# RWKV attention, gated feed-forward and top-2 experts on one core: gate columns computed with the gates as weights in four array quarters, ScalarE's copies and the router's waits in another order

## The chip, the cores and the metric

The kernel runs as one program on one core of a Trainium2 chip. The metric is the time of one execution on the device in microseconds (us), and lower is better. TensorE (PE in the rows) multiplies matrices, VectorE (DVE) and ScalarE (ACT) work on vectors, GpSimd (POOL) issues the indirect transfers and SyncE (SP) nearly all the others. Each engine has its own instruction stream and works it off in order. An engine waits for another by a semaphore.

## What is computed

Three layers in a row, all in fp32:

```python
for t in range(S):                       # B=4, H=8, S=768, D=48
    cur = einsum('bhd,bhe->bhde', u[None] * kt, vt)
    y[:, :, t] = einsum('bhd,bhde->bhe', rt, state + cur)
    state = wt[:, :, :, None] * state + einsum('bhd,bhe->bhde', kt, vt)
x = y.transpose(0, 2, 1, 3).reshape(3072, 384)
x = ((x @ w1) * (x @ w2)) @ w3 @ w_out   # w1, w2: 384x1024, w3: 1024x1024, w_out: 1024x384
noisy = x @ w_gate + log1p(exp(x @ w_noise)) * noise      # 8 experts
top2 = the two largest of noisy; weights = softmax over them
out = sum over the two of weight * (relu(x @ w1[e]) @ w2[e])
```

## The kernel before

Attention goes in chunks of 128 steps; one **pair** is two heads of one batch element, and there are 16 pairs. A pair's steps are: `in` 0 to 2 (PE transposes w, k and r into the tile `tr`, L162; ScalarE copies them out as `wt`, `kt`, `rt`, L232), `derive` (VectorE: running products `decay` L247, their reciprocals L258, `kdiv` L265, `rdec` L271), `diag` (VectorE, L282, L289, L298), `spread` (ScalarE copies the identity, scaled by the diagonal, into `att`, twelve copies of 128x128, L311), `score` (PE L177 into `pp`; VectorE masks it into `att`, L319), `keys` (PE L186, ScalarE L238), `state` (PE L198; VectorE L328 and L333), `scale` (ScalarE makes `state`, L345) and `out` (PE L217 and L223; ScalarE L352). The second `score` needs the mask of the first, since both use `pp`.

The program has four stretches. In the first, the **build** (to 115 us), pairs 0 to 3 run between the steps of a product of weights: `w_out` is transposed (`wo_turn`, L649), its product with the two gate matrices is made (`wo_gates`, L658: 48 records with `woT` as the weights and the 16 gate columns as the moving side), and w3 is transposed block by block (`w3_turn`, L669, ScalarE evacuates to `w3T`, L571) and multiplied with [w_out | gates] (`w3_mm`, L679). ScalarE and VectorE also split w1 and w2 into a high and a low part there (L583, L628), and the products (L586, L614). The second stretch, the **main** one (to 460 us), runs the other 12 pairs between the steps of the feed-forward: `up` (PE L781 into two banks in turn; ScalarE copies one half, `a_sb` L826, VectorE multiplies, `ab_all` L859, then `abh` L822 and `abl` L852; `up` number f+2 needs the `ab_all` of f), `down` (PE L797, ScalarE `x2s` L837), `turn` (the next tokens, `xh` L469 and `xl` L475), and the router: `route` in parts 0 to 3 and `place`, on VectorE with an Exp and a Ln on ScalarE (L843, L845, each Ln and the Exp of `gap`, L848, with an ACT_TABLE_LOAD ahead). The third (to 580 us) ends the feed-forward and starts the experts; the fourth is the experts' visits (L1189, L1205, L1230, L1248), whose code is not touched.

The order of the steps is one list for all engines. `pair_slots` gives ten slots for each pair; `threaded` fills the main steps in behind each slot so that each gets an equal share of the sum of their `LENGTH`s. Each engine runs through that list and issues what it has to do at each step, SP its loads too. In `pair_slots` the copy of the states (`scale`) stands ahead of `in` 0 of the next pair in slot 2, the spreads are two steps of six copies in slots 6 and 7, and `derive` 4 and 5 are in slots 7 and 8.

Before the list starts SP issues a fixed set of loads, among them the second block of w3, `load_w3(1)`.

## Time and profile before

| | us |
|---|---|
| median of three runs | 1058.26 |
| lowest and highest | 1055.92, 1060.39 |
| the profiled execution | 1058.37 |
| its span | 1056.5 |
| PE busy in it | 1018.5 |
| VectorE busy | 706.4 |
| ScalarE busy | 587.4 |

The profiled execution lies 0.11 us above the median, and 1.9 us of its time are outside the span. A row of a timeline is: start, duration, engine, line, operation, what it writes and reads, how many in a row, and in brackets the idle time of the engine before it with what ended it.
### The profile page before, as it was taken

Reading aid. Unit: us, or ns where it says so; the run is one execution under the profiler, and the core shown is the slowest. Engines: PE = TensorE matmul, PEld = TensorE weight load, DVE = VectorE, ACT = ScalarE, POOL = GpSimd, SP = SyncE. Lnnn points to the kernel's source line nnn. Section 1 sums busy time; section 2 is a strip of 40 time slices with the busy share of each in tenths; the row PEclk is TensorE's granted clock in tenths of the full one; section 3 lists DMA queues with packets and bytes.
Section 4 is the critical chain, followed back from the end, with each engine's and each line's share of the span. In section 5 each row is a group of like instructions: output and inputs, shape, how many; then the busy total and the mean of one; then the engine's idle time right before and its main releaser. Section 6 shows DMA issues by size and latency. Waiting matters only on the chain.

```text
span 1056.5 us, 20547 instructions
## 1 busy us (share of the span) xinstructions
PE 1018.5 (96%) x7791; PEld 957.0 (91%) x7791; DVE 706.4 (67%) x1339; ACT 587.4 (56%) x1125; POOL 222.2 (21%) x209
## 2 busy tenths in 40 slices
PE   7999999999999999999998999999999999999995
PEld 6666789989899988999998999999999999999995
DVE  5878567778688677735677658565775857576570
ACT  4655456456456455533564557565664756566471
POOL 0000000110110110111214332343234233323321
PEclk8999999999999999999999999999999999999998
DMA  9654432553634733120557979787888978888851
GB/s 248 168 147 92 105 81 62 84 119 67 88 70 81 119 59 51 43 87 16 185 118 135 270 201 303 208 252 233 237 258 221 291 212 252 247 225 270 225 157 16
DMA packets 190886, 166.41 MB, mean 158 GB/s; under 512 B 118258, under 2 KB 174452, under 8 KB 190788
## 3 DMA queue, kind: packets, MB, share of 16 engines
q1 hardware_dynamic: 177012, 144.76, 50.1%
q0 software_dynamic: 12976, 20.32, 9.8%
q8 instruction: 62, 1.02, 0.4%
q14 instruction: 36, 0.29, 0.1%
q10 hardware_dynamic: 800, 0.02, 0.0%
HBM read 141.21 MB, written 25.22 MB: 158 GB/s over the span
## 4 chain that ended last, share of the span: by engine, by line
PE 90%; ACT 3%; DVE 2%; DMA 2%; issue 1%; POOL 0%; another core or an unknown queue 0%; SPq 0%; DVEq 0%; ACTq 0%; POOLq 0%
PE bank L1189 18%; PE pp L1205 18%; PE bank L781 18%; PE fx L797 10%; PE tr L162 3%; PE yu L1248 3%; PE pp L177 2%; PE yu L223 2%; PE yu L217 2%; PE fx L679 2%; PE bank L679 2%; PE tr L1170 2%; PE yu L1230 1%; PE fx L1230 1%; DMA slot_entry<-entry,slot_i 1%
## 5 line engine op out<-in xcount | busy, mean ns | idle before, releaser
L781 PE MATMUL bank<-xh,w12h 128*128 128x256 f32 x576 | 167.0, 290 | 4.3 <-DVE ab_all L859 3.7
L781 PE MATMUL bank<-xl,w12h 128*128 128x256 f32 x576 | 162.8, 283 | 0.0
L781 PE MATMUL bank<-xh,w12l 128*128 128x256 f32 x576 | 162.7, 282 | 0.0
L1103 POOL DMA_INDIRECT result<-x2s,who x55 | 93.2, 1695 | 275.0 <-ACT x2s L1322 249.9
L1309 DVE SCALAR_TENSOR_TENSOR abl<-bank,abh 128x512 fp32r<-128x512 f32 x96 | 66.2, 690 | 109.9 <-ACT abh L1304 101.7
L958 POOL DMA_INDIRECT slot_entry<-entry,slot_i x48 | 50.0, 1041 | 379.7 <-DVE token_f L947 368.4
L781 PEld LDWEIGHTS bank<-xh,w12h 128*128 128x128 f32 x576 | 110.1, 191 | 7.3 <-DVE ab_all L859 5.0
L781 PEld LDWEIGHTS bank<-xl,w12h 128*128 128x128 f32 x576 | 110.3, 191 | 0.0
L781 PEld LDWEIGHTS bank<-xh,w12l 128*128 128x128 f32 x576 | 110.1, 191 | 0.0
L1189 PE MATMUL bank<-xh,set_up_h 128*128 128x256 f32 x384 | 109.2, 284 | 0.2 <-DVE abl L1309 0.2
L1189 PE MATMUL bank<-xh,set_up_l 128*128 128x256 f32 x384 | 108.6, 283 | 0.0
L1189 PE MATMUL bank<-xl,set_up_h 128*128 128x256 f32 x384 | 108.6, 283 | 0.0
L1304 ACT ACTIVATE abh<-bank 128x512 fp32r<-128x512 f32 x96 | 57.4, 598 | 84.5 <-PE bank L1189 80.6
L859 DVE TENSOR_TENSOR ab_all<-a_sb,bank 128x256 f32<-128x256 f32 x96 | 40.3, 420 | 76.3 <-ACT a_sb L826 71.0
L1205 PE MATMUL pp<-set_down_h,abh 128*128 128x384 f32 x256 | 87.7, 342 | 0.0
L1090 POOL DMA_INDIRECT xr<-ffn_out,who x55 | 74.9, 1362 | 59.0 <-DMA who<-slot_entry 33.2
L1205 PE MATMUL pp<-set_down_h,abl 128*128 128x384 f32 x256 | 85.7, 335 | 0.0
L1205 PE MATMUL pp<-set_down_l,abh 128*128 128x384 f32 x256 | 85.6, 334 | 0.0
L826 ACT COPY a_sb<-bank 128x256 f32<-128x256 f32 x96 | 35.2, 367 | 88.2 <-PE bank L781 84.4
L258 DVE RECIPROCAL kdiv<-decay 128x256 f32<-128x256 f32 x48 | 82.9, 1738 | 0.2
L1322 ACT ACTIVATE x2s<-pp,who 128x384 f32<-128x384 f32 x48 | 27.9, 582 | 85.0 <-PE pp L1205 80.5
L1189 PEld LDWEIGHTS bank<-xh,set_up_h 128*128 128x128 f32 x384 | 73.5, 191 | 0.7 <-DVE abl L1309 0.4
(233 smaller groups left out, 2762.2 us busy)
## 6 DMA issues: line engine op xcount, KB each, us to landing
up_raw<-in_moe_w SPq DMA_DIRECT2D x93, 512.0 KB
down_raw<-in_moe_w SPq DMA_DIRECT2D x124, 384.0 KB
padded<-in_w SPq DMA_DIRECT2D x32, 144.0 KB, 2.8
padded<-in_k SPq DMA_DIRECT2D x32, 144.0 KB
padded<-in_r SPq DMA_DIRECT2D x32, 144.0 KB
vs<-in_v SPq DMA_DIRECT2D x32, 144.0 KB, 3.5
attention_out<-yt SPq DMA_DIRECT2D x64, 72.0 KB, 1.9
xr<-attention_out SPq DMA_DIRECT2D x12, 384.0 KB, 3.7
```

The source lines that it names most:

```text
L258: nc.vector.reciprocal(kdiv[q % 2][:, :].rearrange("p (c x) -> p c x", c=NC)[:, two, :], decay[q % 2][:, two, 1:C + 1]).then_inc(inverse_r ...
L679: last = nc.tensor.matmul(sums[q % 2][:, 0:WA], w3T[q % 2][:, m, :], wo[:, m, :], start=(m == 0), stop=(m == KF - 1))
L781: last = nc.tensor.matmul(bank[f % 2][:, m * TG:(m + 1) * TG], wp[:, m, kk, f * P:(f + 1) * P], xp[:, kk, :], start=(n == 0), stop=(n == 3 ...
L797: last = nc.tensor.matmul(fx[:, 0:WA], xp[:, f, s * P:(s + 1) * P], wp[:, f, :], start=(f == 0 and n == 0), stop=(f == KF - 1 and n == 2))
L859: nc.vector.tensor_tensor(ab[f % 4], a_sb[f % 2][:, :], bank[f % 2][:, TG:2 * TG], ALU.mult).then_inc(ab_free, 1)
L958: nc.gpsimd.indirect_dma_start(slot_entry, bass.IndirectOffsetOnAxis(slot_i[:, s, n:n + 1], 0), entry[:, s, n, :], None).then_inc(scattere ...
L1090: nc.gpsimd.indirect_dma_start(xg[v % 2][:, s, :], None, stored, bass.IndirectOffsetOnAxis(who[v % 4][:, s, 0:1], 0)).then_inc(gathered[v ...
L1103: nc.gpsimd.indirect_dma_start(out, bass.IndirectOffsetOnAxis(who[v % 4][:, s, 0:1], 0), yo[v % 2][:, s, 0:DM], None, bounds_check=N - 1, ...
L1189: last = nc.tensor.matmul(bank[m % 2][:, f * T2:(f + 1) * T2], wp[:, kk, c:c + P], xp[:, kk, :], start=(n == 0), stop=(n == 3 * KD - 1))
L1205: last = nc.tensor.matmul(pp[:, s, 0:DM], xp[:, f, s * P:(s + 1) * P], wp[:, f, :], start=(f == 0 and n == 0), stop=(f == KF - 1 and n == 2))
L1304: nc.scalar.activation(hh[:, 2 * m:2 * m + 2, :].rearrange("p a t -> p (a t)"), bank[m % 2][:, :], ACT.Relu).then_inc(hh_ready, 1)
L1309: nc.vector.scalar_tensor_tensor(hl[:, 2 * m:2 * m + 2, :].rearrange("p a t -> p (a t)"), bank[m % 2][:, :], 0.0, hh[:, 2 * m:2 * m + 2, : ...
```

## The change

1. `wo_gates` becomes one step. The gates, padded with zeros from 16 to 32 columns (a memset on GpSimd, `gates_clear`), are the weights, and `woT` is the moving side, 256 columns at a time: twelve matmuls, three for each quarter of 32 columns of the array. ScalarE copies the 128x256 result into `w3T[1]`, a new step `gates_turn` transposes it back with two transposes on PE, and VectorE copies that into `wo`. In the list `w3_turn` 0,1 stands between the two steps. `LENGTH` gets `gates_turn` 1, while three `wo_gates` of 5 are gone.
2. The spreads are four steps of three copies, at the slots that `SPREAD_AT` names for each pair (5 to 9). The first two parts need only that the first half of the previous output is done. The mask waits for the two parts of its half.
3. In slot 2 `in` 0 stands ahead of `scale`, and `derive` 4 and 5 are both in slot 7.
4. `route` part 0 ends before the wait for the Ln, which goes with its three operations to part 1. The wait for the Exp of `gap`, with the two operations behind it, goes to a part 4, called at the start of `place`.

```diff
+        SPREAD_AT = ((5, 6, 8, 9), (5, 7, 8, 9), (5, 6, 7, 9), (6, 7, 8, 9))
...
-                    [("scale", q, 0), ("in", q + 1, 0)],
+                     [("in", q + 1, 0), ("scale", q, 0)],
...
-                    [("derive", q + 1, 3), ("spread", q + 1, 0)],
-                    [("derive", q + 1, 4), ("spread", q + 1, 1)],
-                    [("derive", q + 1, 5)], []]
+                     [("derive", q + 1, 3)], [("derive", q + 1, 4), ("derive", q + 1, 5)], [], []]
...
-            build += [("wo_gates", n, 0) for n in range(4)] + [("w3_turn", 0, 1)]
+            build += [("wo_gates", 0, 0), ("w3_turn", 0, 1), ("gates_turn", 0, 0)]
...
+                        for kk in range(KD):
+                            for n in range(4):
+                                last = nc.tensor.matmul(fx[4 * E * n:4 * E * (n + 1), 0:2 * P], gates[:, kk, :],
+                                                        woT[:, kk, 2 * P * n:2 * P * (n + 1)],
+                                                        start=(kk == 0), stop=(kk == KD - 1))
...
+                elif part == 1:
                     dve.wait_ge(ln_ready, i + 1)
...
-                else:
+                elif part == 3:
...
-
+                else:
                     dve.wait_ge(exp_ready, 2 * i + 2)
...
             def dve_place(dve, b, q):
 
                 i = NG * b + q
+                dve_route(dve, b, q, 4)
                 dve.wait_ge(place_full, i + 1)
```

PE's instructions at the start, from the transposes of w_out to the first output of pair 0. Before:

```order
L669 MATMUL bank<-ident,w3r 128x128 x4
L162 MATMUL tr<-ident,padded 128x128 x6
L658 MATMUL fx<-gates,woT 128x16 x24
L177 MATMUL pp<-rdec,kdiv 128x128 x6
L186 MATMUL tr<-ident,kdiv 128x128 x5
L669 MATMUL bank<-ident,w3r 128x128 x4
L177 MATMUL pp<-rdec,kdiv 128x128 x6
L198 MATMUL yu<-vs,kend_t 64x48 x10
L669 MATMUL bank<-ident,w3r 128x128 x4
L679 MATMUL fx<-wo,w3T 128x400 x2
```

and of the changed kernel (its L685 is L669 of before, its L695 is L679):

```order
L685 MATMUL bank<-ident,w3r 128x128 x4
L162 MATMUL tr<-ident,padded 128x128 x6
L670 MATMUL fx<-woT,gates 32x256 x12
L685 MATMUL bank<-ident,w3r 128x128 x4
L677 MATMUL fx<-ident,w3T 128x128 x2
L685 MATMUL bank<-ident,w3r 128x128 x4
L695 MATMUL fx<-wo,w3T 128x400 x4
L177 MATMUL pp<-rdec,kdiv 128x128 x6
L186 MATMUL tr<-ident,kdiv 128x128 x5
L177 MATMUL pp<-rdec,kdiv 128x128 x6
L198 MATMUL yu<-vs,kend_t 64x48 x10
```

The first transposes of the second w3 block (the third L685 row) and four matmuls of `w3_mm` moved ahead of the scores L177, and nothing stands between L186 and the second scores.

ScalarE in the build, from the transposed r of pair 2 to its keys. Before:

```order
L232 COPY rt<-tr 128x768
L586 CAST wah<-fx 128x400
L311 ACTIVATE att<-ident,diag 128x128 x12
L571 COPY w3T<-bank 128x512
L583 CAST w12h<-wraw 128x1024
L571 COPY w3T<-bank 128x512
L238 COPY kend_t<-tr 128x640
L586 CAST wah<-bank 128x400
L345 ACTIVATE state<-added,decay 128x48 x5
L232 COPY wt<-tr 128x768
```

and of the changed kernel (L313 is L311, L578 is L571, L593 is L583, L596 is L586, L347 is L345):

```order
L232 COPY rt<-tr 128x768
L313 ACTIVATE att<-ident,diag 128x128 x3
L578 COPY w3T<-bank 128x512
L313 ACTIVATE att<-ident,diag 128x128 x3
L593 CAST w12h<-wraw 128x1024
L313 ACTIVATE att<-ident,diag 128x128 x3
L578 COPY w3T<-bank 128x512
L313 ACTIVATE att<-ident,diag 128x128 x3
L596 CAST wah<-bank 128x400
L238 COPY kend_t<-tr 128x640
```

The first copy out of the w3 transposes now stands behind three spread copies in place of twelve. The copy of `wt` and the states follow a few rows on, with `wt` first.

VectorE in the main stretch, at part 0 of the route of a group. Before:

```order
L258 RECIPROCAL kdiv<-decay 128x256
L886 TENSOR_SCALAR one_z<-exp_z 128x16
L887 SCALAR_TENSOR_TENSOR rest<-one_z,exp_z 128x16
L889 RECIPROCAL noisy<-one_z 128x16
L890 TENSOR_TENSOR rest<-rest,noisy 128x16
L892 TENSOR_TENSOR rest<-ln_z,rest 128x16
L893 TENSOR_TENSOR rest<-rest,noise_all 128x16
L895 TENSOR_TENSOR noisy<-rest,x2s 128x16
L859 TENSOR_TENSOR ab_all<-a_sb,bank 128x256
L852 TENSOR_TENSOR abl<-ab_all,abh 128x256
L265 TENSOR_TENSOR kdiv<-kt,kdiv 128x768
```

and of the changed kernel (L875 is L859, L868 is L852, L909 is L892):

```order
L902 TENSOR_SCALAR one_z<-exp_z 128x16
L903 SCALAR_TENSOR_TENSOR rest<-one_z,exp_z 128x16
L905 RECIPROCAL noisy<-one_z 128x16
L906 TENSOR_TENSOR rest<-rest,noisy 128x16
L875 TENSOR_TENSOR ab_all<-a_sb,bank 128x256
L868 TENSOR_TENSOR abl<-ab_all,abh 128x256
L265 TENSOR_TENSOR kdiv<-kt,kdiv 128x768
L271 TENSOR_TENSOR rdec<-rt,decay 128x768
L875 TENSOR_TENSOR ab_all<-a_sb,bank 128x256
L868 TENSOR_TENSOR abl<-ab_all,abh 128x256
L909 TENSOR_TENSOR rest<-ln_z,rest 128x16
```

The operation that waits for the Ln moved behind two `ab_all`, and `rdec` moved up to `kdiv`.

## Rows read from the trace of the kernel before

**Rows 1.** The page, part 4: the chain that ended last, by engine.
```profile
PE 90%; ACT 3%; DVE 2%; DMA 2%; issue 1%; POOL 0%; another core or an unknown queue 0%; SPq 0%; DVEq 0%; ACTq 0%; POOLq 0%
```

**Rows 2.** What PE waited for: us in total, times, the longest.
```profile
PE tr L162 <- ACT wt L232: 6.0, 6, 1.5
...
PE bank L781 <- DVE ab_all L859: 3.7, 5, 1.0
...
PE pp L177 <- issue: 1.8, 2, 0.9
```

**Rows 3.** Stretches: length, busy time of each engine, PEclk, DMA share, GB/s.
```profile
19.70:26.50 6.80, 6.80 (x40) 6.21 (x40) 1.95 (x3) 1.97 (x5) 0.00 (x0) 0.50 0.91 244
...
67.50:70.90 3.40, 3.40 (x9) 2.03 (x9) 2.79 (x3) 0.69 (x1) 0.00 (x0) 0.50 0.91 239
```

**Rows 4.** The timeline of PE in the first 50 us.
```profile
15.68 6.60 PE L658 MATMUL fx<-gates,woT 128*128 128x16 f32 x48
...
27.77 0.66 PE L669 MATMUL bank<-ident,w3r 128*128 128x128 f32 x4
...
31.61 0.82 PE L162 MATMUL tr<-ident,padded 128*128 128x128 f32 x6
...
32.79 0.65 PE L217 MATMUL yu<-rdec,state 48*64 48x128 f32 x8
33.38 0.88 PE L223 MATMUL yu<-att,vs 128*64 128x128 f32 x12
...
39.83 2.85 PE L679 MATMUL bank<-wo,w3T 128*128 128x400 f32 x8
...
44.39 0.94 PE L177 MATMUL pp<-rdec,kdiv 48*128 48x128 f32 x12
45.26 0.77 PE L186 MATMUL tr<-ident,kdiv 128*128 128x128 f32 x5
...
48.17 0.79 PE L198 MATMUL yu<-vs,kend_t 128*64 128x48 f32 x20
```

**Rows 5.** The load of w3's second block that SP issues at 18.16 us.
```profile
L510 SPq DMA_DIRECT2D w3r<-in_moe_w x1: 542/542/542, 18.2 to 18.2; - x1
...
DMA to landing us min/median/max: 5.4/5.4/5.4
```

**Rows 6.** Timelines of VectorE, ScalarE and PE: the first mask, and pair 2 in the build.
```profile
23.98 1.01 DVE L319 COPY_PREDICATED att<-causal,pp 128x768 f32<-128x768 int32 x1 [1.37 <-PE pp L177]
...
61.82 3.61 ACT L311 ACTIVATE att<-ident,diag 128x128 f32<-128x128 f32 x12
...
65.96 0.66 PE L669 MATMUL bank<-ident,w3r 128*128 128x128 f32 x4 [1.43 <-ACT w3T L571]
```

**Rows 7.** The timeline in the main stretch where states stand ahead of `wt`.
```profile
211.37 1.49 ACT L345 ACTIVATE state<-added,decay 128x48 f32<-128x48 f32 x5 [1.80 <-DVE added L328]
...
212.77 0.78 ACT L232 COPY wt<-tr 128x768 f32<-128x768 f32 x1
...
213.69 0.85 PE L162 MATMUL tr<-ident,padded 128*128 128x128 f32 x6 [1.45 <-ACT wt L232]
...
216.62 0.65 PE L217 MATMUL yu<-rdec,state 48*64 48x128 f32 x8
```

**Rows 8.** The timeline at the Ln of a route, second batch element.
```profile
286.72 1.75 DVE L258 RECIPROCAL kdiv<-decay 128x256 f32<-128x256 f32 x1
...
288.20 1.28 ACT L845 ACT_TABLE_LOAD   x1
...
289.82 0.18 DVE L892 TENSOR_TENSOR rest<-ln_z,rest 128x16 f32<-128x16 f32 x1 [0.62 <-ACT ln_z L845]
...
290.92 0.39 PE L781 MATMUL bank<-xh,w12h 128*128 128x256 f32 x1 [1.00 <-DVE ab_all L859]
```

**Rows 9.** The timeline of VectorE behind the Exp of `gap`.
```profile
260.40 0.17 DVE L920 TENSOR_SCALAR total<-exp_gap 128x2 f32<-128x2 f32 x1 [0.68 <-ACT exp_gap L848]
...
261.48 0.95 DVE L271 TENSOR_TENSOR rdec<-rt,decay 128x768 f32<-128x768 f32 x1
```

**Rows 10.** The chain that ended last, around the scatter of the last but one group.
```profile
554.61 12.37 DMA slot_entry<-entry,slot_i
```

More of the change, by code:

```diff
@@ L576, in first_act @@
                         evacuate(q)
+                    elif step == "wo_gates":
+                        act.wait_ge(gates_full, 1)
+                        nc.scalar.copy(w3T[1][:, 0:2, :].rearrange("p n f -> p (n f)"), fx[:, 0:2 * P]).then_inc(gates_out, 1)
                     elif step == "w3_turn":
```

67 lines of the change are left out of this document (37 added, 30 removed).

## The prediction

> **What bounds the kernel now.** I read the chain that ended last first: PE carries 90% of it [rows 1]. So only three things count: work that leaves PE, idle time of PE, and time at the low clock. The list of what PE waited for gives the second: 6.0 us for ScalarE's copy of `wt` in six places, 3.7 us for `ab_all`, 1.8 us at the scores [rows 2]. The stretches give the third: from 19.7 to 26.5 and from 67.5 to 70.9 us PE was granted 0.50 and was busy all the time [rows 3]. The first of these began inside the gate step, 48 records in 6.6 us [rows 4].
>
> **The gate step and the start.** The change takes 48 records away that are paced by their loads of weights. In their place come 24 records of 256 columns and two transposes. No row shows four quarters. Two halves are in the trace: twelve records of 128 columns in 0.88 us [rows 4], 0.073 us each, so 0.147 for 256 columns and 3.5 us for 24. Without any overlap a record costs what the full array needs: 2.85 us for eight of 400 columns [rows 4], 0.89 ns a column, 5.5 us in all. With all four quarters beside each other it is near 1.4 us. So PE is done with the gates between 17.1 and 21.2 us, and behind `w3_turn` 0,1 and the transposes between 18.4 and 22.3. None of this reaches the end. The next steps in the list are now the transposes of w3's second block. SP issues its load at 18.16 us and it lands 5.4 us later, at 23.6 [rows 5]; the order of SP up to there is not changed, and its queue is full of earlier loads. Before, these transposes ran at 27.77 [rows 4] and met no wait. Now PE stands still 1 to 5 us in front of them, and the scores, which need nothing from that load, are queued behind.
>
> What is left from 23.6 on: before, from 27.77 to 32.79 us is 5.0 us [rows 4], of which two transposes of inputs (0.82 us each, 0.65 from start to start) don't count, since they come later in the new list as well: 3.7. Added are two scores, the keys and the state products, 0.94 + 0.94 + 0.77 + 0.79 [rows 4], 3.1 us with their overlaps. Nothing stands any more between the keys and the second scores, so these wait for the mask of the first: 1.01 us [rows 6] and 0.2 to start it, less the 0.6 of the keys, 0.6 us. Together 7.4 us, which ends at 31.0. The same point of before is 32.79 - 1.3 = 31.5. At full clock the start gains 0.5 us.
>
> But the clock. In the build an idle of 1.43 us [rows 6] and the light work behind it were followed by 3.4 us at 0.50 [rows 3]. I take one such piece behind the new, longer idle: 3.4 us at half rate lose 1.7. The start then **loses 1.2 us**. Bounds: a gain of 0.5 if the gates run without overlap, the idle is short and the clock stays; a loss of 2.9 if the low piece is as long as the first one, 6.8 us [rows 3].
>
> The Trainium skill has a rule that speaks against this change (TensorE: Matmul & The Clock Gate, "HAM oscillation — how this bites in real kernels"): if the array has to wait for a transfer between two stretches of matmuls, it is throttled and begins the next stretch cold. By that rule the wait for w3 costs a cold stretch; without it my sum would be 1.7 us lower. The trace agrees as far as it goes, with an idle that a copy caused and not a transfer.
>
> **Spreads in four parts.** In pair 2 the copy out of the w3 transposes stands behind twelve spread copies of 3.61 us [rows 6]. In the new order it stands behind three, 0.9 us. PE's idle of 1.43 us goes, and with it the low piece behind it, 1.7 us: **-3.1 us**. What is late next is VectorE: by my count of the steps it has some 12 us of work from `wt` to `rdec`, and PE 13 to 14 us between the same two points, so it fits, with about 1 us to spare. One of the build's pairs gets the keys and second scores side by side, which costs 0.6 us for the mask as above: **+0.6**.
>
> **`wt` ahead of the states.** ScalarE waited 1.80 us for VectorE's `added` and then made the states, 1.49 us; the `wt` copy came behind and PE idled 1.45 us for it [rows 7]. Now the copy starts when its transposes have ended, and these stand ahead of VectorE's work on the states; it is done before PE wants `tr`. All six waits go: **-6.0 us** [rows 2]. The states are up to 0.8 us later. The output that reads them starts at 216.62 [rows 7], 3.8 us behind the last state; that covers it. The bound is -3: in the build the shares between steps are short, and a wait may come back there.
>
> **The route's waits.** In three places PE idled 1.00 us for `ab_all` [rows 8]. The chain there: reciprocal of 1.75 us on VectorE, `one_z` behind it, ScalarE's table load of 1.28 us and Ln, `a_sb`, and VectorE's wait of 0.62 for the Ln with three small operations, before `ab_all` [rows 8]. The new order takes the Ln's wait and the three operations (0.6 us) away, and three of the six spread copies in front of the Exp. I work the new times out: reciprocal to 288.5, `one_z` to 288.6, Ln to 288.8, `a_sb` to 289.1, `ab_all` to 289.8. PE wants it at 289.92. So the idle just goes, with 0.1 us to spare: -3.0, and -0.2 in the last route: **-3.2 us**. Where the last spread part now stands right in front of the Exp, the next `up` but one comes 4 us later, behind the scores, so nothing waits.
>
> `rdec` at 261.48 [rows 9] came behind the wait for the Exp of `gap`, and the scores waited 0.9 us for it, twice [rows 2]. It now follows `kdiv` at once and ends 2 us earlier: **-1.8 us**. The gap, its Exp and the following `ab_all` are 0.6 us later, behind a `down` that has 1.7 us in hand.
>
> In the last groups two operations (0.4 us) are now part of `place`, ahead of the scatter whose transfer of 12.37 us is in the chain [rows 10]. The late table hangs on it, and PE is idle behind that table: **+0.4 us**. In the other groups nothing waits for `place`. From 580 us on the code and the order are the same, and I expect the same time. GpSimd's memset of the gates lies beside the first loads, at no cost.
>
> **Sum.** Against the profiled execution, 1058.4: -6.0 - 3.1 - 3.2 - 1.8 = -14.1; +1.2 + 0.6 + 0.4 = +2.2. That is -11.9: **1046.5 us**. The profiled execution stands at the median, so I take the same for the median.
>
> **The rivals.**
> *B: the waits of the route come back in another form.* My margin at the Ln is 0.1 us, and the reciprocal in front of `one_z` stays where it is. For it: VectorE has next to no idle time in such a group. Against it: the spread copies in front are halved. If half a microsecond more is late in each of the places, and the states or VectorE give back as much as one wait for each batch element, 4 to 5 us of the gain stay away: 1051.
> *C: the start and the build take more back.* The low piece is 6.8 us long (+1.7), and VectorE's margin of under 1 us in the build breaks in two or three pairs (+2), on top of half of B (+2.3): 1052.5 to 1054, within half a per cent of before.
> *D: slower than before.* One mechanism: after the wait for w3 the clock stays low through the build, because the small waits for masks there keep it from rising. Work at half rate costs 0.5 us for each us. The gains outside the start are 13.1 - 0.4 us or so; from some 25 us of low clock on, up to about 49 us in the run, it is a loss. If it lasts through the 90 us of the build, +45 - 13: 1090. Against it: before, the clock rose again inside 7 us each time [rows 3], among work as light as this.
> That the change doesn't do what it says is true for its first part in my forecast already: the gate columns are shorter on PE and the end doesn't see it.
>
> **How the numbers follow.** Forecast 0.63, its own range 1043.5 to 1049 (the start from -0.5 to +2.9 in place of +1.2, the finale's 0.4 or not, a build wait more or less). B 0.19 at 1051, C 0.13 at 1053, D 0.05. The range that holds 8 in 10 reaches over B: 1043 to 1054. A difference of 0.5%, 5.3 us, is about what a measurement of this kernel can tell from no change; faster than 1053.0 are the forecast, B and half of C: 0.88; within it 0.07; slower 0.05.
>
> **What would show it.** PE idle 1 to 5 us in front of the third w3 transposes, ending near 23.6 us, and PEclk at 0.50 behind it. No wait for `wt`, none for `w3T` behind spreads, no low clock near 68 us. The wait of VectorE for the Ln gone, `rdec` straight behind `kdiv`. The main stretch some 8 us shorter, the build from 30 us on some 4. I am wrong if PE has no idle near 20 us (then the start gains 1 to 3 us more), if the idle of 1.00 us is still there three times, or if PE waits for state copies, `kend_t` or masks in the main stretch.

## The result, and the profile after

The changed kernel takes **1053.2 us** in the median of 19 runs (1049.5 to 1056.0), beside 1060.0 for the kernel before on the same chip (19 runs): a ratio of **0.9938**, 95% interval 0.9925 to 0.9951. The medians are 6.8 us apart where 11.9 were forecast. Three more comparisons, one on chip 1 and two on chip 2, gave 0.9921, 0.9959 and 0.9968. Lines have moved by 16 below the diff, and by 17 behind `place`: L781 is now L797, L797 is L813, L810 is L826, L669 is L685, L1189 is L1206.

What PE waited for in the changed kernel, without the first load of all and the rows under 1.1 us (us in total, times, the longest), from its profiled execution of 1054.0 us:

```profile
PE bank L685 <- DMA w3r<-in_moe_w: 5.3, 1, 5.3
...
PE yu L223 <- issue: 3.4, 1, 3.4
PE fx L813 <- ACT x2s L853: 3.1, 8, 0.7
PE bank L1206 <- DVE abl L1326: 2.5, 2, 2.0
PE tr L162 <- ACT wt L232: 1.2, 2, 0.6
PE bank L826 <- DVE abl L1326: 1.1, 1, 1.1
PE bank L797 <- DVE ab_all L875: 1.1, 1, 1.1
```

Against [rows 2], `wt` fell from 6.0 to 1.2 us, the route's waits at `ab_all` from 3.7 to 1.1 (that one is in the last groups), and the 1.8 us at the scores are gone. Of the long rows two are new. The first is the wait for w3's second block, as forecast. This is the timeline of PE there:

```profile
15.11 1.50 PE L670 MATMUL fx<-woT,gates 128*32 128x256 f32 x24
16.55 0.66 PE L685 MATMUL bank<-ident,w3r 128*128 128x128 f32 x4
17.11 0.44 PE L677 MATMUL fx<-ident,w3T 128*128 128x128 f32 x2
22.90 1.12 PE L685 MATMUL bank<-ident,w3r 128*128 128x128 f32 x4 [5.35 <-DMA w3r<-in_moe_w]
```

The second is in no step of the prediction. In the middle of twelve output matmuls PE stands for 3.39 us. No semaphore, no engine and no transfer of the program releases it:

```profile
390.79 0.87 PE L217 MATMUL yu<-rdec,state 48*64 48x128 f32 x12
391.60 0.87 PE L223 MATMUL yu<-att,vs 128*64 128x128 f32 x11
395.86 0.31 PE L223 MATMUL yu<-att,vs 128*64 128x128 f32 x1 [3.39 <-issue]
396.10 0.88 PE L162 MATMUL tr<-ident,padded 128*128 128x128 f32 x6
```

Around both idles PE was granted half clock: from 21.54 us, while it still stood, and from 397.00 us. The stretches (length, busy time of PE, PEld, DVE, ACT, POOL with their instructions, PEclk, DMA share, GB/s):

```profile
21.54:28.36 6.82, 5.46 (x11) 3.28 (x12) 0.00 (x0) 3.28 (x8) 0.00 (x0) 0.50 0.66 211
397.00:400.40 3.40, 3.40 (x18) 3.40 (x18) 1.77 (x2) 1.68 (x5) 0.00 (x0) 0.50 0.77 216
```

The up matmuls start 0.21 us apart in the second stretch and 0.12 at full clock, so up to half of its 3.4 us is lost. This one event cost some 3.39 + 1.7 = 5.1 us, an estimate. The up product's matmuls give a scale: in the traces the first begins at 115.9 us before and 114.3 after. The stretch from there to the last one I call the main stretch: 424.4 us before, 421.4 after, and without the event it would be 416.3. At the up matmul that starts at 388.8 us the changed kernel was 9.1 us ahead; at the one that starts at 401.8 it was 3.9 ahead.

### The profile page after: what moved, and what is told of

It is laid out like the page before. It is cut to its first block, busy times and chain, and to the rows that moved or that the text cites. A ratio compares the mean times of both kernels' runs of the same rounds, so it can differ in the third digit from the quotient of the medians.

```text
span 1052.2 us, 20504 instructions
## 1 busy us (share of the span) xinstructions
PE 1013.2 (96%) x7769; PEld 951.2 (90%) x7769; DVE 705.6 (67%) x1339; ACT 584.3 (56%) x1126; POOL 221.7 (21%) x210
## 4 chain that ended last, share of the span: by engine, by line
PE 90%; DVE 4%; ACT 2%; SPq 2%; issue 1%; DMA 0%; POOL 0%; another core or an unknown queue 0%; DVEq 0%; ACTq 0%; POOLq 0%
PE pp L1222 19%; PE bank L1206 19%; PE bank L797 19%; PE fx L813 9%; PE tr L162 3%; PE yu L1265 3%; PE fx L695 2%; PE pp L177 2%; PE yu L223 2%; PE bank L695 2%; PE yu L217 2%; PE tr L1187 2%; PE yu L1247 1%; PE fx L1247 1%; PE yu L198 1%
## 5 line engine op out<-in xcount | busy, mean ns | idle before, releaser
L797 PE MATMUL bank<-xh,w12h 128*128 128x256 f32 x576 | 167.8, 291 | 1.7 <-DVE ab_all L875 1.1
L797 PE MATMUL bank<-xl,w12h 128*128 128x256 f32 x576 | 163.5, 284 | 0.0
L797 PE MATMUL bank<-xh,w12l 128*128 128x256 f32 x576 | 163.4, 284 | 0.0
L797 PEld LDWEIGHTS bank<-xh,w12h 128*128 128x128 f32 x576 | 110.8, 192 | 4.5 <-DVE ab_all L875 2.0
L797 PEld LDWEIGHTS bank<-xl,w12h 128*128 128x128 f32 x576 | 110.9, 193 | 0.0
L797 PEld LDWEIGHTS bank<-xh,w12l 128*128 128x128 f32 x576 | 110.8, 192 | 0.0
L1206 PE MATMUL bank<-xh,set_up_h 128*128 128x256 f32 x384 | 109.2, 284 | 0.0
L1206 PE MATMUL bank<-xl,set_up_h 128*128 128x256 f32 x384 | 108.6, 283 | 0.0
L1206 PE MATMUL bank<-xh,set_up_l 128*128 128x256 f32 x384 | 108.6, 283 | 0.0
L875 DVE TENSOR_TENSOR ab_all<-a_sb,bank 128x256 f32<-128x256 f32 x96 | 40.3, 420 | 84.6 <-ACT a_sb L842 80.1
L1206 PEld LDWEIGHTS bank<-xh,set_up_h 128*128 128x128 f32 x384 | 73.5, 191 | 0.5 <-DVE abl L1326 0.2
```

What stands on the lines that cost most here:

```text
L797: last = nc.tensor.matmul(bank[f % 2][:, m * TG:(m + 1) * TG], wp[:, m, kk, f * P:(f + 1) * P], xp[:, kk, :], start=(n == 0), stop=(n == 3 ...
L875: nc.vector.tensor_tensor(ab[f % 4], a_sb[f % 2][:, :], bank[f % 2][:, TG:2 * TG], ALU.mult).then_inc(ab_free, 1)
L1206: last = nc.tensor.matmul(bank[m % 2][:, f * T2:(f + 1) * T2], wp[:, kk, c:c + P], xp[:, kk, :], start=(n == 0), stop=(n == 3 * KD - 1))
```

## The experiments

All edits are against the changed kernel unless said otherwise. Each group of kernels ran beside the kernel before on one chip; its median lay between 1054.5 and 1071.5 us from chip to chip, so ratios are compared and not times. The groups were: e1 to e4 on chip 2; e5, e6, e8 and e9 on chip 14; e11 to e14 on chip 10; e15 to e18 on chip 1; e19 and e20 on chip 2. The changed kernel itself was in the first, fourth and fifth group, with ratios from 0.9921 to 0.9968, so on chips 14 and 10 a ratio inside that band says no more than "about the changed kernel". An "idle by issue" is one of PE that nothing releases; the times given for it are where it begins or ends. Such rows at the scores (L177, near 262 and 381 us) are left out of the counts, since there PE waits for `rdec`. Each kernel has one trace, of one execution.

### A second trace, and the parts undone one at a time

> The changed kernel unaltered, for a second trace and as the yardstick of the three beside it. Its first trace holds one thing that no step of the prediction has: at 392.47 us TensorE stands for 3.39 us in the middle of twelve output matmuls (L223, no wait of their own, nothing else of the core running), and its clock is at half for the 3.4 us after, some 5.2 us in all. Theory: that is not a wait of the program but an event of one execution; the second trace then has no idle of more than 1.5 us at L223 at that place, the main stretch alone is some 8 us shorter than in the kernel before, and the profiled span lies 3 to 5 us under the first trace's 1052.2. Rival: it belongs to how the program now lies against its transfers at this place, and shows again within 2 us of 392.5 us with 2 to 4 us. Time either way 1051 to 1054 us.

Ratio 0.9921 (0.9893 to 0.9949). The idle is there again, at the same last L223, with 1.78 us from 398.95 us on, and a second one of 1.62 us at 242.3. First up product 115.1, main stretch 428.4. **The rival's reason holds**, that it comes back in this program. Its numbers do not: it named 2 to 4 us within 2 us of 392.5. The traced execution took 1065.7 us, 4.6 above the median of its kernel.

```
-build += [("wo_gates", 0, 0), ("w3_turn", 0, 1), ("gates_turn", 0, 0)]
+build += [("wo_gates", n, 0) for n in range(4)] + [("w3_turn", 0, 1)]
```

> The changed kernel with the gates' product as before (48 matmuls of 16 columns, no turn, no second copy), all else changed. Theory: the 5.1 us that the matmuls are quicker are eaten by the wait for w3's second block (5.35 us in the trace after), so this kernel has the 6.6 us product again, hardly any wait behind it, and takes 0 to 1.5 us less than the changed one at the same place: about the same time, 1050.5 to 1053.5 us. Rival: with everything behind it the quicker product still gains, as the title of the change suggests, and this one is 2 to 4 us slower, 1055 to 1057 us.

First up product at 112.1 us, against 114.3 to 115.1 in the changed kernel's traces: at this point **the gates' part loses 2.2 to 3.0 us**. In the end it is 3.5 us over e1 (ratio 0.9951, 0.9922 to 0.9981), which is the rival's time. But the rival's reason isn't there. The main stretch is 429.6 us, 1.2 more than e1's, with idles by issue of 1.59, 1.35 and 2.00 us, and the traced span is 0.9 us shorter than e1's. So the traces do not show where the 3.5 us between the medians come from. The theory is right on the start, where it named too little, and wrong on the time.

```
-at = [ROUTE * i + (0, 4, 10, 11, 13)[part]]
+at = [ROUTE * i + (0, 7, 10, 11)[part]]
```

> The changed kernel with the route's wait for the logarithm back at the end of its first part and the sum and reciprocal back in its fourth; no other part undone. Theory by the prediction's sum: three idles of 1.00 us ahead of the up matmuls come back, and the two of 0.89 us ahead of L177: 3 to 5 us slower than the changed kernel, 1056 to 1058 us, and the idles at the down matmuls (0.65 us x2) and in the finale (1.08 and 1.12 us), which the trace after has and the one before has not, go. Rival: those new idles are the same time moved, and the whole is within 1.5 us of the changed kernel, 1052 to 1054.5 us.

Ratio 1.0051 (1.0017 to 1.0084), 11.6 us over e1: far more than either. The waits that came back are small: 1.3 us at the up matmuls in three places, and nothing at the scores. The wait at the place matmul fell from 1.1 to 0.4 us. The trace has idles by issue of 3.34 us at L223 (278 us) and 6.00 us (400 us), and 10.2 us at half clock in the main stretch. Its span is only 4.1 us over e1's, though, so most of the 11.6 us is in no trace and stays open.

```
-[("in", q + 1, 0), ("scale", q, 0)]
+[("scale", q, 0), ("in", q + 1, 0)]
```

> The changed kernel with ScalarE's two steps in the third slot of a pair back in the old order (states evacuated ahead of the first of the next pair's three inputs), nothing else undone. Theory by the prediction's sum: the three idles of 1.35 to 1.45 us and the one of 0.97 us ahead of L162 come back in its trace, and with them 4 to 6 us from the start to the last up matmul; its time is 3 to 6 us over the changed kernel's, a ratio to the kernel before of 0.996 to 1.000. Rival: the evacuation now stands behind a shorter piece of ScalarE's work, so that it comes back at 0.5 us each only, a ratio of 0.991 to 0.995.

Ratio 0.993 (0.9897 to 0.9962): the rival's. `wt` is waited for 4.1 us in four places instead of 1.2 in two, and PE has 5.7 us of idles by issue in the main stretch. The traces of the changed kernel beside others have 1.2 us (e19), 1.8 (e16) and 2.2 (e1) for `wt`.

```
-SPREAD_AT = ((5, 6, 8, 9), (5, 7, 8, 9), (5, 6, 7, 9), (6, 7, 8, 9))
+SPREAD_AT = ((6, 6, 7, 7),) * 4      # "derive" 5 back in its own slot
```

> The changed kernel with the diagonal copies in their old slots (all twelve in two neighbouring slots, the last derivation behind them). Theory by the prediction's sum: the idle of 1.43 us ahead of the last wo_turn's neighbour in the build and 1.7 us of half clock behind it come back (in the trace after, no half clock stands between 30 and 390 us), so it is 2 to 3.5 us slower than the changed kernel by the first up matmul, and 0 to 1 us more in the main stretch: a ratio to the kernel before of 0.995 to 0.998. Rival: with states behind inputs the copies hide anyway, and the ratio is that of the changed kernel, 0.991 to 0.995.

Ratio 0.9944 (0.9917 to 0.9971), the rival's, and yet the copies don't hide. The first up product begins at 114.8 us, as in the changed kernel, and no idle of 1.43 us is in the build. What comes back is in the main stretch:

```profile
PE tr L162 <- ACT wt L232: 6.2, 5, 1.8
...
PE bank L797 <- DVE ab_all L875: 4.2, 4, 2.3
```

At the scores 1.5 us come back as well, in the two places where PE waited for `rdec`: the edit puts `derive` 5 back too, so this trace does not tell the copies from that. What it does show is that the `wt` term hung on these slots as much as on the states. Undoing either alone brings a part of it back.

### The wait for w3

```
-for n in range(3):
-    sp_input_load(sp, 0, 1, n)
 load_w3(1)
+for n in range(3):
+    sp_input_load(sp, 0, 1, n)
```

> The changed kernel with one queue entry moved: the load of w3's second block is issued ahead of the three input loads of the second head pair, at about 12.9 us in place of 18.17 us. Theory: the block lands at 17.5 to 19 us instead of 22.8, the idle of 5.35 us ahead of the next turn falls below 1.5 us, and the gain of 4 to 5 us is kept to the end of the build: 1047.5 to 1050 us. Rival: the time comes back at once, since the second pair's inputs now land later, the chain of scores and states sets the pace of the start, and the first up matmul starts within 1 us of where it does in the changed kernel (114.3 us): 1052 to 1053.5 us.

Ratio 0.9852 (0.981 to 0.9894), 6.7 us under e1. The wait is 1.18 us and the clock stays whole:

```profile
19.27 0.66 PE L685 MATMUL bank<-ident,w3r 128*128 128x128 f32 x4 [1.18 <-DMA w3r<-in_moe_w]
```

```profile
19.00:107.00 88.00, 85.56 (x643) 57.65 (x644) 67.70 (x100) 53.70 (x132) 1.00 (x14) 1.00 0.65 160
```

The first up product is at 108.0 us, 6.3 to 7.1 us sooner. That is 4.2 us of idle and about 3 us of the half clock's loss, and the inputs that land later take nothing of it back.

> The same kernel as e4_w3_early (w3's second block loaded ahead of the second pair's inputs), for a second trace, on another chip if it comes so, and as the yardstick of the one beside it. Theory: its gain over the changed kernel (6.7 us on one chip) is of the program: a ratio to the kernel before of 0.983 to 0.989, the first up product 5 to 7 us sooner than in the changed kernel, and no piece of half clock ahead of 100 us, as in its first trace. Rival: part of it was that trace's luck with the clock (10.2 us at half in the changed kernel's start against none): the half clock comes back, and the ratio is 0.988 to 0.993.

Ratio 0.9884 (0.9868 to 0.9901), first up product 107.5, no half clock ahead of 277 us. The clock and the place are the theory's; the ratio lies in both ranges. The expectation gives the changed kernel 10.2 us at half clock in the start; its trace has 6.8.

> w3's second block loaded ahead of the second pair's inputs and the gates' product as before, all else changed: e4_w3_early without the gates' part. Theory: once the block is early, the wait no longer eats the 5.1 us that the new gates' matmuls save, so without them the first up product is 3 to 6 us later than in e4 (107 to 108 us) and the ratio to the kernel before is 0.990 to 0.993. Rival: with the gates' product long, the load was early enough anyway and something else sets the start: first up product within 1.5 us of e4's, the gates' part being worth nothing even then.

First up product at 111.7 us against 107.4 to 108.8 in the five traces with the early load and the new gates. **With the block early, the gates' part gains 2.9 to 4.3 us; with it late, it loses 2.2 to 3.0.** A part of that is the clock: with the old gates PE was granted half clock for 10.2 us from 18 us on, in e2 and in e17, and in none of the five. Early loading alone, with the old gates, is worth 0.4 us (112.1 to 111.7), one trace each on two chips. Ratio 0.9932 (0.9906 to 0.9958), just above the theory's range.

### The idles by issue

These rows are stretches from 0 to the end of such an idle. Behind the length come PE and PEld, and the numbers in brackets count their records: matmuls and loads of weights. First e16, the changed kernel again, up to an idle near 209 us:

```profile
0.00:212.20 212.20, 192.04 (x1575) 154.49 (x1576) 147.76 (x266) 111.64 (x274) 8.30 (x56) 0.99 0.53 123
```

And e17, which like the kernel before has the old gates and so 44 records more in the build:

```profile
0.00:206.07 206.07, 195.20 (x1579) 159.88 (x1580) 146.13 (x263) 110.94 (x271) 8.23 (x55) 0.98 0.52 125
```

Nine traces have one here, all behind 3145 to 3161 records and ending between 202 and 212 us, that of e15 (the kernel before, 0.77 us) among them. The work at that count is not the same, as PE's rows of e16 and then of e17 show:

```profile
212.22 0.37 PE L797 MATMUL bank<-xh,w12l 128*128 128x256 f32 x1 [3.70 <-issue]
```

```profile
206.09 0.70 PE L198 MATMUL yu<-vs,kend_t 128*64 128x48 f32 x7 [2.28 <-issue]
```

The second place, in the first trace of the changed kernel, then in e3 and in e8:

```profile
0.00:395.84 395.84, 374.60 (x3211) 323.71 (x3211) 292.26 (x639) 212.18 (x534) 28.19 (x76) 0.99 0.50 107
```

```profile
0.00:406.42 406.42, 377.19 (x3212) 325.03 (x3213) 292.47 (x639) 212.29 (x534) 27.72 (x76) 0.98 0.52 104
```

```profile
0.00:410.54 410.54, 378.58 (x3211) 325.92 (x3212) 292.12 (x639) 211.30 (x534) 28.20 (x76) 0.98 0.46 103
```

Eight of the fifteen traces with the changed kernel's stream of matmuls have an idle here, behind 6422 to 6425 records. It ends between 392 and 411 us and takes 0.85 to 6.66 us. So the same place of the program comes again at other times. **The first place is no step of the work, the second can't be told.** At one step of the work the old gates would have 44 records more, 3189 to 3201; they have 3151 to 3161. By time they are not apart: they end at 205.8 to 208.6 us, the others at 202.7 to 212.2. At the second place all eight traces have one stream, in which count and step are the same. Against a pure count there stand the four traces with the old gates, which have none behind 6422 to 6425 records. e17 stands for 3.84 us behind 6520 instead, its longest idle by issue:

```profile
400.64 0.57 PE L787 MATMUL bank<-xh,w12l 128*128 128x256 f32 x1 [3.84 <-issue]
```

One thing that would come at fixed counts of the stream is the code itself. The page of the changed kernel shows a queue for it, with packets, MB and share:

```profile
q8 instruction: 62, 1.02, 0.5%
```

That is 16 KB a packet, one for each 251 of the 15,538 records of PE. The Trainium skill (Runtime: NRT & Kernel Launch, "Instruction fetch mechanics") says that an engine's instructions are streamed in blocks of 16 KiB, 256 instructions each, over a DMA queue of its own, and calls the cost mostly hidden. The size agrees with the trace. Whether these idles are that cost, no run here shows directly. The packets of q8 next to the idle of 3.39 us are at 378.9 and 398.2 us, and none is seen to end with it. One idle of all the traces does end with such a packet: in e9 a packet starts at 282.18 us and takes 10.63 us, and PE, idle for 2.39 us, goes on at 292.94, 0.13 us behind its end.

> The changed kernel with 40 matmuls of 16 columns that nothing uses, put where TensorE waits for w3's second block, so that the code behind lies 80 instructions further on in TensorE's stream while its work lies at the same times. In the changed kernel's stream (four kernels of that stream) TensorE stood at the same instruction, the last of the twelve L223 near 392 to 400 us or one of the five right behind it, for 1.3 to 6.0 us, whatever the time was. Theory: it waits there for the next piece of its own code, fetched by transfers that are slow at that time, and the piece ends at a fixed count of instructions; here the idle moves 40 matmuls up in the work, to an up matmul some 5 us before that L223, where the stretch is just beginning, and is under 1.5 us or gone. Rival: the wait belongs to that instruction or to that time: again 1.5 us or more at L223 or L162 at 392 to 401 us. Time within 4 us of the changed kernel's either way; if the theory holds, rather below: ratio to before 0.986 to 0.993.

The edit was dearer than meant: a matmul counts as two records of each kind, so the stream moved by 160, and the 80 matmul records took 13.8 us in the place of an idle of 5.35. First up product at 123.2, ratio 1.0039 (1.0004 to 1.0074). There is no idle at either old count, nor at the last L223. Others stand elsewhere: they end at 252.9 (1.28 us), 292.9 (2.39), 338.3 (1.99) and 417.9 us (1.94), the last behind that L223 and not ahead of it. Where it would go was forecast wrongly. More than that the run does not show: seven of the fifteen traces of the unshifted stream have no idle at that L223 either, so one trace without it speaks neither for the count nor against the instruction.

> The changed kernel, unaltered, as the yardstick of the one beside it. So far its stream of TensorE instructions stood without a release at two counts of matmul and weight-load records from the program's start: 3234 to 3246 (near 201 to 212 us) and 6578 to 6582 (near 391 to 410 us). Theory (the counts are where a new piece of its code has to be in): every idle by issue of over 1.2 us in the main stretch stands at one of those two counts or at one seen in the same stream before (3775, 4455 to 4535, 5256). Rival: they fall anywhere. Ratio to the kernel before 0.992 to 0.996.

Ratio 0.9968 (0.9942 to 0.9994). The idles are behind 3151 records (0.99 us) and behind 6423 (0.85), with a second of 0.86 three matmul records further on, and no other reaches 0.5 us. That suits the forecast but doesn't test it, since it spoke of idles over 1.2 us and there is none. The expectation counts the same two places as 3234 to 3246 and 6578 to 6582; the rows above give 3145 to 3161 and 6422 to 6425.

> The changed kernel, unaltered, beside e15 on one chip. Theory: on a quiet chip its trace holds no idle of over 1.2 us that nothing releases, the main stretch gains 7 to 8 us against either trace of before, and what is missing of the gain lies in the start: first up product at 114 to 115 us. Rival: the idle at the last L223 near 392 us is there with 1.3 us or more on this chip too. Ratio to the kernel before 0.992 to 0.996.

Ratio 0.9959 (0.9942 to 0.9977). Neither as expected: nothing at L223, but 3.70 us at the first count. Main stretch 420.2 us, of which 5.4 are that idle and the half clock behind it.

### What is slow at that time

The idles at the second place fall in stretches in which transfers hardly move. Here are 388 to 396 us of the changed kernel, and 396 to 402 of the kernel before (packets of the queue that carries all direct transfers, MB, its time as a share of 16 engines):

```profile
DMA packets 966, 0.19 MB, mean 24 GB/s; under 512 B 958, under 2 KB 966, under 8 KB 966
...
q1 hardware_dynamic: 966, 0.19, 106.2%
```

```profile
DMA packets 1066, 0.26 MB, mean 43 GB/s; under 512 B 1023, under 2 KB 1066, under 8 KB 1066
...
q1 hardware_dynamic: 1066, 0.26, 104.4%
```

All 16 engines are taken in both, and a packet is slower in the changed kernel: 0.14 us in the mean against 0.09. Not every packet is slow: the median of the packets of 192 bytes is 15 ns in both stretches.

This isn't so for all idles. At the first place the engines were busy for 0.06 of the time in e4's idle (201.4 to 202.7 us) and for 0.16 in e17's (203.8 to 206.1). **In e2 PE stood for 2.00 us, from 323.5 to 325.5, in a stretch from 318 to 326 us in which the trace has no DMA packet at all.** Slow transfers can't be the cause of that one, and no packet of q8 lands there.

SyncE's queue shows what has moved together. First the changed kernel:

```profile
386.34 1.04 SPq L137 DMA_DIRECT2D padded<-in_w  x2
389.13 0.79 SPq L153 DMA_DIRECT2D attention_out<-yt  x2
389.97 0.55 SPq L773 DMA_DIRECT2D result<-zeros  x1
```

And the kernel before:

```profile
394.15 1.03 SPq L137 DMA_DIRECT2D padded<-in_w  x2
399.75 0.79 SPq L153 DMA_DIRECT2D attention_out<-yt  x2
400.59 0.55 SPq L757 DMA_DIRECT2D result<-zeros  x1
```

From the input load to the attention store are 5.6 us before (3.9 in e15), and 2.8 to 3.1 in the four traces of the changed kernel. It is 3.1 also in e11 to e14, all on the quickest chip, and none of these stands at that L223; in e12 the store lands as late as here, after 8.2 us, and PE does not stand. So the collision alone doesn't bring the idle. In the kernel before PE's wait of 1.35 us for `wt` lay between them; without it the store comes on top of the load. The store lands after 4.3 us before and 8.3 in the changed kernel's first trace. e6, where the `wt` waits are back, has 4.5 us between the two and no idle by issue over 0.75 us.

```
 if step == "down" and n == 5:
-    sp_group_store(sp, b, q)
+    held.append((b, q))               # stored behind the next ("out", *, 1)
```

> The changed kernel with SyncE's store of a finished group (ffn_out<-x2s, 384 KB) held back until behind the next load of values, some 10 us later, where no input load follows for 9 us. In all traces so far a stretch in which packets of 192 bytes take 100 to 500 ns in place of 15 begins within 1 us of an input load that is issued right behind this store (near 235, 275, 355 and 395 us), and all but a few of TensorE's idles that nothing releases (1.2 to 6.0 us, five kernels) lie in or at the end of such a stretch. Theory: the store colliding with the loads is the cause; here the slow stretches shrink to below half, TensorE's idles by issue of over 1 us go, and the kernel takes 3 to 8 us less than the changed one on the same chip: a ratio to the kernel before of 0.984 to 0.989. Rival: the loads and the attention stores are slow by themselves, or the late store slows other transfers instead: ratio 0.991 to 0.996, with stretches as before at other places.

Ratio 0.9964 (0.9936 to 0.9992). **The theory fell.** The packets of 192 bytes are quick (29 ns in the mean from 401 to 407 us), those of the attention store, of 1536 bytes, take 1.2 us in the mean instead, and PE stands 6.66 us behind 6423 records, the longest idle of all.

```
+if i < GROUPS - NG:
+    pool.wait_ge(ab_full, KF * (i + 2) + 1)
 for s in range(ST):                   # the four scatters
```

> The changed kernel with GpSimd's scatters of a group (slot_entry<-entry, four a group) held until the first up product of the group after the next, some 10 us later, for the first six of the nine groups. The group store is not the cause: with it held back the packets of 192 bytes were quick, but those of 1536 bytes (attention stores) took 1.3 to 3 us each from 401 to 407 us, and TensorE stood 6.66 us at the same instruction. In all traces the slow stretches begin 2 to 6 us behind the last scatter. Theory: the scatters bring them on; here they lie about 10 us later, away from 388 to 404 us, and TensorE's idle at the last L223 of that place is under 1 us. Rival: they belong to the third input load, the attention stores and the clearing of the result, which stand together whatever the scatters do: slow packets and an idle of 1.3 us or more at 390 to 405 us again. Time: 2 to 5 us under the changed kernel's on the same chip if the theory holds, within 2 us if not.

Ratio 0.9942 (0.9926 to 0.9959), inside the changed kernel's band. The trace has no idle by issue of 0.5 us or more in the main stretch, the stretch at 390 us is quick, and slow packets lie at 208 to 213 and 284 to 287 us. This was on the quickest of the chips, though, where the kernel before takes 1054.5 us.

```
-sp.dma_start(out[part * rows:(part + 1) * rows, :]...   # 384 KB
+sp.dma_start(out[part:part + 1, :]...                   # one row
```

> The changed kernel without the clearing of the result: each of its stores of zeros (384 KB, seven or eight of them from 190 to 480 us) writes one row instead, so the rows of the result that are added to start from what the memory holds. What it tells is the time of the main stretch. Theory: it is this store, issued 0.8 us behind the attention stores, that fills the queues while TensorE's next code is being fetched: the idle at the last L223 near 392 to 404 us and its like (1.2 to 6.7 us) go, the stretch from the first to the last up product is 2 to 6 us shorter than the changed kernel's. Rival: the slow packets begin ahead of that store (in the trace after at 387.5 us, the store at 389.97), so its absence changes nothing of them: idle of 1.3 us or more there again, time within 2 us of the changed kernel's.

Ratio 0.9956 (0.9934 to 0.9978). The kernel leaves out the clearing, so its result is not the right one; what counts is its time. Slow packets as before at 388 to 396 us: the rival is right that the clearing doesn't make them. No idle by issue all the same, and a main stretch of 417.7 us; whether that is the edit or the chip, which is e11's, isn't told apart.

```
-if n == 0:
+if n == 1:
     sp_clear(sp, HP * b + q)          # on top of e4's edit
```

> e13_w3_again with the clearing of the result issued behind the second half's attention store and the values' load in place of between the two halves. Theory: the queues are then free for the code and the stores in the stretch where TensorE stood, and the ratio to the kernel before is 0.003 to 0.006 below e13's. Rival: it collides there with the next inputs' load instead, and the ratio is within 0.002 of e13's or above it.

Ratio 0.9874 (0.9857 to 0.989), within 0.002 of e13's, so the rival. Its trace is the shortest of all: first up product 107.4, main stretch 414.0 with no idle by issue, span 1039.7. The slow stretch is there all the same, from 383 to 387 us.

> e14_w3_clear_late a second time (w3's second block ahead of the second pair's inputs, the clearing of the result behind the values' load), beside the changed kernel on one chip. Theory: 6 to 9 us faster than the changed kernel, first up product 6.5 to 7.5 us sooner, ratio to the kernel before 0.985 to 0.990, and idles by issue that sum to less than the changed kernel's. Rival: on another chip the second edit is worth nothing and the ratio is 0.990 to 0.993.

Beside the changed kernel on one chip: 1054.2 us against 1063.2, **9.0 us faster**, ratio to the kernel before 0.9876 (0.9837 to 0.9916). The time is the theory's, though the first up product is only 5.8 us sooner. The idles by issue are more than the changed kernel's, 1.78 us and, behind 6424 records, 5.42, against 2.70 in e19, where the theory had less. So the late clearing doesn't cure them; e14 ran on the chip that hardly has them.

> e14_w3_clear_late with the scatters held back as in e11 too. In e11's trace the slow stretch of 388 to 404 us was gone and TensorE had no idle by issue in the main stretch, in e14's two slow stretches were left with no idle. Theory: the slow transfers stretch lies where the scatters put it, and away from everything it costs nothing: ratio to the kernel before 0.982 to 0.987, no idle by issue over 1 us in the main stretch. Rival: e14 has nothing left to gain there: ratio within 0.002 of 0.9874.

Ratio 0.9928 (0.9902 to 0.9954), worse than e13 and e14 on theirs. An idle by issue of 1.99 us is behind 3157 records, and PE waits 2.98 us at the down matmuls at 508 us. The theory fails.

> The kernel before, unaltered, for a second trace. Its first trace has no idle of TensorE that nothing releases from 120 to 540 us, the changed kernel's first has one of 3.39 us, and on a chip where the changed kernel with the scatters held back shows none, it was still only 6.0 us faster than the kernel before in the median, though its trace lies 9.8 us under the first trace of before. Theory: the kernel before varies too, and the first trace of it was slow at the start by its half clock (10.2 us at half in two pieces): some executions have fewer of these. This trace then shows half clock of 3.4 us or none in the start and a first up product 1.5 to 4 us sooner than 115.9 us, or all steps alike and a span 2 to 4 us shorter for other reasons that it names. Rival: the trace is like the first to within 1 us up to 540 us, and the difference lies in the visits behind.

Ratio to itself 1.0004 (0.9986 to 1.0021). The second trace of the kernel before has its first up product at 114.8 and a main stretch of 423.0 us. PE waits for `wt` 3.2 us in four places, where the first trace has 6.0 in six:

```profile
PE tr L162 <- ACT wt L232: 3.2, 4, 1.4
PE bank L781 <- DVE ab_all L859: 3.0, 3, 1.0
PE pp L177 <- issue: 2.8, 2, 1.4
```

The idle of 1.43 us at L669 in the build is there too, and no half clock follows it. Of the two low pieces of the first trace one, of 3.4 us, is missing and one of 6.8 stays, where the theory had 3.4 or none. The start is 1.1 us shorter in place of 1.5 to 4, and the main stretch differs as well, which the rival didn't have.

## Why the prediction fell short, point by point

The direction was right, and the time lies inside the wide range (1043 to 1054), at its edge. It lies outside the forecast's own, 1043.5 to 1049. The size was not right: 6.8 us where 11.9 were forecast. **The step that failed is the sum over the main stretch.** It took 6.0, 3.2 and 1.8 us of waits as time that simply goes, with no new idle in their place. The waits nearly all went, and the main stretch became 3.0 us shorter instead of 8, because PE stood for 2.7 to 3.7 us in new places, with 3.4 us or more at half clock behind (between e15 and e16, on one chip, it became 2.8 us shorter). Two further terms were off, the start and the copies.

**The gates and the start: right in mechanism, a loss of 2.2 to 3.0 instead of 1.2.** PE's idle in front of w3's second block was forecast as 1 to 5 us ending near 23.6; it was 5.35 us ending at 22.90. The gates ran in 1.50 us, which is the value for four quarters beside each other. I had bounded the clock with 3.4 us at half and taken that; it was 6.8 us, the upper bound, in three of the changed kernel's four traces, and 3.4 in e16. That the half clock began while PE still stood makes its cost less than half of 6.8: PE was busy for 5.46 us of it, an estimated loss of 2.7.

**The copies in four parts: the term was wrong.** -3.1 was made of an idle of 1.43 us and of 1.7 for the clock. The second trace of before has the idle without the low clock. In e6 the first up product comes no later (114.8 us, against 114.3 to 115.1). What worth the copies have lies in the main stretch, where they stood ahead of `wt` copies, and e6 doesn't separate it from that of `derive` 5.

**`wt` ahead of the states: the waits went, 4.8 of 6.0 us.** Two of 0.60 us stayed in the build, and 1.2 to 2.2 us in all stayed in the four traces. But 6.0 was one trace's value, another has 3.2, and the term shares its cause with the copies. To add both, from one profile, counts a part twice.

**The route and `rdec`: right in what went, not in who took it away.** The three idles of 1.00 us and the 1.8 us at the scores are gone, and where 0.1 us of margin was forecast nothing came back as `ab_all`. But the route alone undone (e3) gave only 1.3 of the 3.0 us back and nothing at the scores, and e6 gave 1.9 and 1.5 us. So the copies' slots carry a share of the first and `derive` 5's slot most of the second. At the down matmuls (`x2s`, L813) the wait grew from 2.3 to 3.1 us, a small piece of rival B.

**The finale: +0.4 forecast.** The wait at the place matmul (L826) is 1.1 us in all traces of the changed kernel and 0.4 before, 0.7 more, and e3 has 0.4 again.

**The step that is missing.** The main stretch was to be some 8 us shorter. In e11's trace, with no idle by issue, it is: 415.8 against 424.4 us, though that kernel has an edit more and no trace of the changed kernel is without idles. In the four traces of the changed kernel PE stands 2.7 to 3.7 us for no release, with 3.4 us or more at half clock behind it. The two traces of before have none and 0.77 us of it. **By this subtraction some 4 to 5 us of the gain were made and then lost again there.** I had costed each wait as time that simply goes, and I didn't ask what else could stop PE in the shorter stretch. Why it stands there is not shown.

Of the rivals, C names the right time (1053), in part by luck: its low piece of 6.8 us came, while VectorE's margin in the build held and of the route's waits only 0.8 us came back. D didn't happen: each low piece ended within 6.8 us.

What is open: the cause of the idles. That PE waits for its code is one reading. For it are the size of the blocks, that the instructions around wait for nothing, the one idle of e9 that ends with a packet of q8, and that in five of the eight traces the next packet of q8 starts within 0.9 to 2.3 us of the end of the idle at the second place. Against it are the idle of e2 in a stretch without any packet, and that no other ends with one. Which transfer makes the slow stretches is not settled: not the group store and not the clearing; the scatters may have a share, but e11 and e18 ran on different chips and speak for and against. And the idles alone don't explain why before, on the quickest chip, has a median 4 us under its first trace, nor the 11.6 us of e3.

**A version that beats both** is e13 with or without the later clearing: 0.9874 to 0.9884 of before on one chip, 0.9852 and 0.9876 on another, where the changed kernel had 0.9921 and 0.9968 beside them.

## What to carry to other kernels

When an edit makes one stretch of an engine quicker, look first at what the next instruction in its order waits for. Here the quicker gates ran into a load that one line in SyncE's order could issue 5 us sooner, and only both together gained. Take a second trace before adding waits up: two of the terms were one execution's. A trace also need not stand for its kernel: e1's execution lay 4.6 us over the median. And before calling a place a count, look for streams in which the count and the work come apart.

## What the runs showed of the hardware

- PE can stand for 0.77 to 6.66 us in a run of matmuls that wait for nothing, and often at the same place of the program in execution after execution (behind 6422 to 6425 records in eight traces, 3145 to 3161 in nine). Most of those over 1.3 us in the main stretch had 3.4 to 10.2 us of half clock around or behind them; four (1.35, 1.62, 1.78 and 1.99 us) had none. One of 2.00 us (e2) stands in 8 us without any DMA packet.
- A stretch of 966 packets, 958 of them under 512 bytes, took 8 us of all 16 engines: 24 GB/s. Its packets of 192 bytes took 136 ns in the mean, with a median of 15 ns; from 140 to 160 us the mean is 16.
- Twenty-four records of 256 columns in four quarters of the array took 1.50 us, 62 ns a record; two halves before took 73 ns for 128 columns.
- The same idle of 1.43 us (e15 and the first trace of before) was followed by half clock in one execution and not in another.
